# Attention, MLP and mixture of experts on one core: power-of-two scales in fewer links, and VectorE's work reordered around the weight scales, the first rows and the third gate chunk

## The chip, the core and the metric

The kernel runs on one core of a Trainium2 chip. The metric is the device time in microseconds (us) of that launch; the time of a kernel is the median of its runs.

## What is computed

```python
def phi(x):                                    # q, k: (4, 8, 576, 64), w_phi: (64, 128)
    proj = x @ w_phi
    proj = proj - max(abs(proj), axis=-1)
    return concat([exp(proj), exp(-proj)])     # 256 features
kv  = phi(k)^T @ v ;  z = sum over s of phi(k)
att = (phi(q) @ kv) / (phi(q) @ z + 1e-6)      # -> x: (2304, 512)
h = x @ w_in                                   # (512, 2048)
x = (h * clip(h + 3, 0, 6) / 6) @ w_out        # (2048, 512)
e = argmax(x @ w_gate)                         # 8 experts, one per row
out = softmax(x @ w_gate)[e] * sigmoid(x @ w_output_gate)[e] * (relu(x @ w1[e]) @ w2[e])   # (512, 1024, 512)
```

All inputs and outputs are fp32. The big products of the MLP and of the experts are made of fp16 parts: a matrix is scaled by a power of two, its high part is rounded to fp16, and its low part is what is left. Three matmuls (high*high, high*low, low*high) stand for one product. The power of two comes from the largest magnitude: its exponent bits are kept, the rest is masked away.

## The kernel before

The program is written engine by engine, with semaphores by hand. Each engine runs its own list in order, so a wait holds up all that stands behind it on that engine.

**Stage 1, attention (about 2.7 to 196 us).** The 32 heads are worked off as 16 pairs, u = 0 to 15. For each pair TensorE (PE) projects q and k in three groups (`projections`, L738, groups g0 of 4 matmuls, g1 and g2 of 16), VectorE (DVE) takes the maxima and the differences (`differences`, L1278, L1280, L1284), ScalarE (ACT) makes the exponentials (`k_features` L1088, `q_features` L1073), GpSimd (POOL) sums k's features (`sums_first` L587 three times, `sums_second` L587 and L603) and multiplies the result of an older pair by its reciprocals (`normalise`, L607), and PE makes kv (L766), z (L786), the numerators (L794) and the denominators (L803). A projection group of pair u+1 may only begin when `differences` has read the bank that it writes: g1 of pair u+2 waits for `differences(u+2, a, 0)`, g2 for `differences(.., 1)`.

DVE's list of a pair is `both(u, a, phase)`. Between the steps of the attention it does side work: `v_max` (L1312, largest magnitude of v of pair u+2), and, one eighth of w_in and of w_out per pair, in pairs 0 to 7 the search for the maximum (`piece_max_of`, L1317) and in pairs 8 to 15 the split (`piece_lo_of`: L1326 the high part of w_in, L1328 the low part of either; ACT's `piece_hi_of`, L1133, the high part of w_out).

**The two special pairs.** In pair 7 (`weights_pair`) the maxima of w_in, w_out and the gate weights are brought together: DVE reduces them (L1361, L1363), PE turns them over the partitions (`max_turn`, L810), DVE reduces again (L1344) and writes the result over a row (L1345, `s_rows`), and PE spreads it to all partitions (`max_over`, L814). Then `scales` makes the exponent, the reciprocal, the scale and its inverse (L1354 to L1357), each a link that waits for the one before. In pair 14 (`values_pair`) the same is done with the maximum of v for the rows x; then `first_x` writes the high part (L1439) and `x_lo` the low part (L1444) of the first 384 rows. DVE's list ends there with `piece_lo_of(14, 0, 1)`, the low part of a piece of w_out, and PE's first MLP block waits for it (`piece_lo`), beside `xs_lo` (the low part of the rows).

**Stage 2, MLP (197.5 to 584 us).** The 2304 rows go in 6 blocks of 384, each over 16 chunks f of the hidden width. PE: `hidden(n, a, f)` (12 matmuls, L878) runs two chunks ahead of `output(n, f)` (9 matmuls, L889). For each chunk ACT makes relu (L1216), DVE the product (`gate_chunk`, L1592), ACT the high part (L1227), DVE the low part (`gate_lo`, L1597); `output` waits for the low part. Where f is in SOON = (0, 1, 15), `gate_lo` stands right behind `gate_chunk`; else it is the last step of the chunk, behind the side work. The side work on DVE: 16 units of the experts' weights are searched (L1509), scaled (`unit_scale`, L1525 to L1529) and split (`unit_lo`, L1536), three units per block, and the rows of the block before are scaled (`row_scales` L1473 to L1482, `row_units` L1494 and L1495, `rows_lo` L1501) and routed.

**Stage 3, experts (584 to 850 us).** 27 slots of 128 rows: hidden (L972) and output (L984) on PE.

## Time and profile before

| | |
|---|---|
| time, median of 3 runs | 849.37 us (847.5 to 850.06) |
| the profiled execution, its own time | 852.16 us |
| span of the profiled execution | 850.5 us |
| busy: PE / DVE / ACT / POOL | 811.7 / 569.2 / 388.1 / 182.5 us |
| mean granted TensorE clock | 0.99 |

The span runs from the first to the last instruction of the profiled execution. Busy time of PE is modelled from pipelined matmuls, so a busy PE may still be waiting a little. Times of instructions below are microseconds from the start of the span.

### The profile page before, as it was taken

The numbers are of one execution on the slowest core, as the hardware profiler recorded it, in microseconds if no ns is written. First come the engines' busy times: TensorE is split into PE (matmuls) and PEld (weight loads), VectorE is DVE, ScalarE is ACT, GpSimd is POOL, SyncE is SP. The second block draws the span as 40 slices with busy tenths as digits, with TensorE's granted clock in tenths as the row PEclk, the third lists the DMA queues.
The fourth block names the chain that finished last, engine by engine and source line by source line (L and its number), as shares of the span: only waits on it lengthen the run. The fifth ranks groups of instructions, "written<-read, shape, count | busy, mean of one in ns | idle before, by whom it ended". The sixth has DMA issues, their size and how long they took to land.

```text
span 850.5 us, 19326 instructions
## 1 busy us (share of the span) xinstructions
PE 811.7 (95%) x7110; PEld 509.4 (60%) x7111; DVE 569.2 (67%) x1149; ACT 388.1 (46%) x841; POOL 182.5 (21%) x211
## 2 busy tenths in 40 slices
PE   6999999999999999999999999999889999999995
PEld 5666666665554554554555455556657777777773
DVE  4777878898988898897998998845622453222221
ACT  5777668884555646646546555524001121111110
POOL 4446547762000001001001001010220222111100
PEclk9999989999999999999999999999999999999998
DMA  7456647856564864955764855584171852556610
GB/s 229 150 186 206 201 139 226 234 160 212 198 243 149 241 238 162 267 205 187 243 225 185 247 209 210 150 293 178 51 278 47 322 207 84 222 225 218 222 69 14
DMA packets 67454, 164.41 MB, mean 193 GB/s; under 512 B 28615, under 2 KB 32967, under 8 KB 60737
## 3 DMA queue, kind: packets, MB, share of 16 engines
q1 hardware_dynamic: 61472, 146.74, 51.5%
q0 software_dynamic: 5760, 16.80, 5.7%
q8 instruction: 36, 0.59, 0.3%
q14 instruction: 26, 0.20, 0.1%
q10 hardware_dynamic: 160, 0.07, 0.0%
HBM read 114.16 MB, written 47.55 MB: 190 GB/s over the span
## 4 chain that ended last, share of the span: by engine, by line
PE 61%; DVE 23%; issue 8%; DMA 3%; ACT 2%; another core or an unknown queue 1%; DVEq 0%; POOL 0%; SPq 0%; ACTq 0%; POOLq 0%
PE ps L984 13%; PE ps L889 12%; PE ps L972 12%; PE ps L878 12%; DVE arena L1536 4%; PE ps L738 3%; DVE u_mx L1509 3%; DVE arena L1278 2%; PE ps L766 2%; PE ps L794 2%; DVE relu L1592 2%; DMA arena<-split 2%; PE ps L962 1%; DVE y_words L1501 1%; PE ps L752 1%
## 5 line engine op out<-in xcount | busy, mean ns | idle before, releaser
L878 PE MATMUL ps<-arena,w_in_sb 128*128 128x384 f16 x1152 | 200.9, 326 | 1.9 <-DVE w_out_sb L1328 1.9
L889 PE MATMUL ps<-w_out_sb,arena 128*128 128x512 f16 x576 | 171.3, 379 | 5.8 <-DVE stage L1597 5.8
L878 PEld LDWEIGHTS ps<-arena,w_in_sb 128*128 128x128 f16 x1152 | 111.9, 98 | 83.0 <-issue 2.1
L972 PE MATMUL ps<-x_t,arena 128*128 128x128 f16 x2112 | 121.5, 219 | 5.9 <-issue 5.9
L1255 ACT ACTIVATE x_t<-ps 128x512 f16<-128x512 f32 x54 | 31.6, 596 | 207.0 <-PE ps L972 176.1
L972 PEld LDWEIGHTS ps<-x_t,arena 128*128 128x128 f16 x2112 | 119.1, 98 | 10.2 <-issue 7.0
L984 PE MATMUL ps<-arena,x_t 128*128 128x512 f16 x528 | 118.0, 379 | 2.5 <-DVE x_t L1702 2.5
L889 PE MATMUL ps<-w_out_sb,stage 128*128 128x512 f16 x288 | 109.1, 379 | 0.0
L1227 ACT ACTIVATE arena<-relu 128x384 f16<-128x384 f32 x96 | 50.0, 521 | 114.1 <-DVE relu L1592 114.1
L1088 ACT ACTIVATE arena<-ps,arena 128x128 f32<-128x128 f32 x288 | 79.9, 393 | 34.8 <-DVE arena L1280 27.8
L889 PEld LDWEIGHTS ps<-w_out_sb,arena 128*128 128x128 f16 x576 | 55.6, 98 | 67.0 <-issue 8.6
L1702 DVE SCALAR_TENSOR_TENSOR x_t<-ps,x_t 128x512 f16<-128x512 f32 x54 | 36.7, 689 | 85.6 <-ACT x_t L1255 85.6
L1216 ACT ACTIVATE relu<-ps,three,s_h 128x384 f32<-128x384 f32 x96 | 63.7, 663 | 56.7 <-PE ps L878 55.2
L984 PEld LDWEIGHTS ps<-arena,x_t 128*128 128x128 f16 x528 | 50.5, 98 | 59.4 <-ACT x_t L1255 2.9
L1536 DVE SCALAR_TENSOR_TENSOR arena<-arena,u_up 128x1024 f16<-128x1024 f32 x64 | 79.3, 1280 | 6.3 <-ACT arena L1204 5.6
L587 POOL TENSOR_TENSOR arena<-arena 128x512 f32<-128x512 f32 (+1 forms) x64 | 64.5, 1008 | 71.8 <-ACT arena L1088 67.3
L1204 ACT ACTIVATE arena<-arena,u_up 128x1024 f16<-128x1024 f32 x64 | 72.5, 1140 | 6.5 <-DVE u_up L1528 6.3
L1509 DVE TENSOR_REDUCE u_mx<-arena 128x1 f32<-128x1024 f32 x64 | 74.8, 1210 | 0.0
L636 POOL PARTITION_ALL_REDUCE u_all<-u_red x16 | 7.6, 476 | 307.1 <-DVE u_red L1513 307.1
L1592 DVE SCALAR_TENSOR_TENSOR relu<-relu,ps 128x384 f32<-128x384 f32 x96 | 52.7, 549 | 26.1 <-ACT relu L1216 24.4
L1278 DVE TENSOR_REDUCE arena<-ps 128x8 f32<-128x1024 f32 (+1 forms) x48 | 45.8, 954 | 35.5 <-PE ps L738 35.3
L1712 DVE TENSOR_SCALAR x_t<-ps,stage 128x512 f32<-128x512 f32 x27 | 20.2, 748 | 70.0 <-PE ps L984 70.0
(208 smaller groups left out, 931.0 us busy)
## 6 DMA issues: line engine op xcount, KB each, us to landing
arena<-split SPq DMA_DIRECT2D x36, 1024.0 KB
arena<-in_moe_w SPq DMA_DIRECT2D x16, 2048.0 KB
split<-arena SPq DMA_DIRECT2D x16, 2048.0 KB, 7.4
arena<-in_qkt SPq DMA_DIRECT2D x15, 576.0 KB, 6.7
stage<-in_moe_w_in SPq DMA_DIRECT2D x16, 512.0 KB, 5.3
stage<-in_moe_w_out SPq DMA_DIRECT2D x16, 512.0 KB, 6.5
x_t<-rows POOLq DMA_DIRECT2D x27, 257.0 KB, 3.0
y_words<-recs SPq DMA_DIRECT2D x32, 144.0 KB, 3.1
```

Of the source, the lines that this page charges most:

```text
L587: nc.gpsimd.tensor_tensor(out, x, y, ALU.add).then_inc(sum_step, 1)
L878: last = nc.tensor.matmul(ps[:, HB[f % GB], 0:BN], w_in_sb[:, lw, c, f * P:(f + 1) * P], xt[:, a, lx, c, :], start=c == 0 and lw + lx == 0 ...
L889: last = nc.tensor.matmul(ps[:, YB + r, :], g_sb[lg_][:, f % GB, r * P:(r + 1) * P], w_out_sb[:, lw, f, :], start=f == 0 and lg_ + lw == 0 ...
L972: last = nc.tensor.matmul(ps[:, bank, f % 4 * P:(f % 4 + 1) * P], w1_sb[b][:, lw, c, f * P:(f + 1) * P], xgt[:, a, lx, c, :], start=c == 0 ...
L984: last = nc.tensor.matmul(ps[:, 6 + a, :], hg[:, a, lh, f, :], w2_sb[b][:, lw, f, :], start=f == 0 and lh + lw == 0, stop=f == EFC - 1 and ...
L1088: last = nc.scalar.activation(pk[:, t0 + t, s, :], ps[:, bank, t * F:(t + 1) * F], ACT.Exp, bias=bias[:, t0 + t:t0 + t + 1], scale=1.0 - 2 ...
L1204: nc.scalar.activation(split_sb[:, 0, q_ * Q:(q_ + 1) * Q], raw[b][:, q_ * Q:(q_ + 1) * Q], ACT.Copy, scale=u_up[:, b:b + 1]).then_inc(u_h ...
L1216: nc.scalar.activation(relu3[:, f % GB, :], ps[:, HB[f % GB], 0:BN], ACT.Relu, bias=three[:, 0:1], scale=s_h[:, 0:1]).then_inc(relu3_ready, 1)
L1278: nc.vector.tensor_reduce(mx[:, j:j + 2, t0:t0 + n], src, AX.X, ALU.max, apply_absolute_value=True).then_inc(max_ready, 1)
L1509: nc.vector.tensor_reduce(u_mx[:, q_:q_ + 1], raw[b][:, q_ * Q:(q_ + 1) * Q], AX.X, ALU.max, apply_absolute_value=True).then_inc(u_searche ...
L1536: nc.vector.scalar_tensor_tensor(out=split_sb[:, 1, cols], in0=raw[b][:, cols], scalar=u_up[:, b:b + 1], in1=split_sb[:, 0, cols], op0=ALU ...
L1592: nc.vector.scalar_tensor_tensor(out=relu3[:, f % GB, :], in0=relu3[:, f % GB, :], scalar=6.0, in1=ps[:, HB[f % GB], 0:BN], op0=ALU.min, o ...
```

## The change

- **Scales in three links.** `scales`, `row_scales` and `unit_scale` made the power of two in clamp, mask, reciprocal, multiply (and inverse). Now they mask, then clamp and multiply to the inverse scale in one instruction, then take its reciprocal as the scale. The inverse scales hold the factor that was multiplied in later, so two later multiplications (that of `slot_inv` for the early slots, and L1783) become a copy or nothing.
- **No spread row.** The copy to `s_rows` (L1345) is gone; PE reads `s_row` as a broadcast.
- **The maxima pair.** In `weights_pair` the gate weights' maximum is taken first, the search of the w_out piece moves behind `differences(u + 1, 1 - a, 1)`, and `scales` comes ahead of `v_max`, which moves behind `differences(u + 2, a, 0)`. In `both`, `v_max` also moves behind `differences(u + 2, a, 0)`.
- **First rows.** In `values_pair`, `first_x` comes ahead of the steps to `s_h` and `s_y` (`x_units`). PE's first block no longer waits for the last piece of w_out (a semaphore of its own, `piece_lo_out`). POOL's last two `normalise` wait for `xs_lo`.
- **MLP blocks.** SOON also holds 2. `row_units` moves from f = 0 to f = 4.

```diff
-USTEPS = 5
+USTEPS = 4
-SOON = (0, 1, FC - 1)
+SOON = (0, 1, 2, FC - 1)
...
             def last_pair():
                 sums_second(PAIRS - 1)
+                pool.wait_ge(xs_lo, 1)
                 for u in range(PAIRS - 1 - BEHIND, PAIRS - LAST):
                     normalise(u, u % 2)
...
                     pe.wait_ge(piece_hi, PAIRS // 2 - 1)
-                    pe.wait_ge(piece_hi_out, PAIRS // 2 - 1)
                     pe.wait_ge(piece_lo, PAIRS // 2 - 1)
+                    pe.wait_ge(piece_hi_out, PAIRS // 2 - 2)
+                    pe.wait_ge(piece_lo_out, PAIRS // 2 - 2)
...
             def max_over_rows(k, n):
                 dve.wait_ge(max_turned, k + 1)
-                scaled(nc.vector.tensor_reduce(s_row[0:n, :], ps[0:n, KVB, 0:P], AX.X, ALU.max))
-                nc.vector.tensor_copy(s_rows[0:n, :], s_row[0:n, :].to_broadcast([n, P])).then_inc(max_spread, 1)
+                nc.vector.tensor_reduce(s_row[0:n, :], ps[0:n, KVB, 0:P], AX.X, ALU.max).then_inc(max_spread, 1)
 
             def max_of(k, cols):
                 dve.wait_ge(num_done, TOPS[k] + 1)
-                scaled(nc.vector.tensor_scalar(s_max[:, cols], ps[:, NB + 1, MAX_AT:MAX_AT + (cols.stop - cols.start)], TINY, None, ALU.max))
+                top = ps[:, NB + 1, MAX_AT:MAX_AT + (cols.stop - cols.start)]
+                scaled(nc.vector.tensor_scalar(s_pow[:, cols].bitcast(I32), top.bitcast(I32), EXPONENT, None, ALU.bitwise_and))
 
             def scales(cols):
-                scaled(nc.vector.tensor_scalar(s_pow[:, cols].bitcast(I32), s_max[:, cols].bitcast(I32), EXPONENT, None, ALU.bitwise_and))
-                scaled(nc.vector.reciprocal(s_up[:, cols], s_pow[:, cols]))
-                scaled(nc.vector.tensor_scalar(s_up[:, cols], s_up[:, cols], 2.0 ** TOP, None, ALU.mult))
-                scaled(nc.vector.tensor_scalar(s_inv[:, cols], s_pow[:, cols], 2.0 ** -TOP, None, ALU.mult))
+                scaled(nc.vector.tensor_scalar(s_inv[:, cols], s_pow[:, cols], TINY, 2.0 ** -TOP, ALU.max, ALU.mult))
+                scaled(nc.vector.reciprocal(s_up[:, cols], s_inv[:, cols]))
...
             def both(u, a, phase):
                 differences(u + 1, 1 - a, 2)
                 pair_out(u, a)
-                v_max(u + 2, a)
                 piece(u, a, 1)
                 differences(u + 2, a, 0)
+                v_max(u + 2, a)
 
             def weights_pair():
                 u, a = TOPS[0], 1
-                for w in range(2):
-                    piece_max_of(u, a, w)
+                gate_max()
+                piece_max_of(u, a, 0)
+                differences(u + 1, 1 - a, 1)
+                piece_max_of(u, a, 1)
                 weight_max()
-                differences(u + 1, 1 - a, 1)
                 max_over_rows(0, 3)
                 differences(u + 1, 1 - a, 2)
                 max_of(0, slice(0, 3))
                 pair_out(u, a)
+                scales(slice(0, 3))
+                differences(u + 2, a, 0)
                 v_max(u + 2, a)
-                weight_scales()
-                differences(u + 2, a, 0)
...
                 pair_out(u, a)
-                x_scales()
+                scales(slice(3, 4))
                 first_x()
+                x_units()
                 piece_lo_of(u, a, 1)
...
-                link(nc.vector.tensor_scalar(y_mx[:], y_mx[:], TINY, None, ALU.max))
                 link(nc.vector.tensor_scalar(y_pow[:].bitcast(I32), y_mx[:].bitcast(I32), EXPONENT, None, ALU.bitwise_and))
-                link(nc.vector.reciprocal(y_up[:], y_pow[:]))
-                link(nc.vector.tensor_scalar(y_up[:], y_up[:], 2.0 ** ETOP, None, ALU.mult))
+                link(nc.vector.tensor_scalar(y_inv[:], y_pow[:], TINY, 2.0 ** -ETOP, ALU.max, ALU.mult))
+                link(nc.vector.reciprocal(y_up[:], y_inv[:]))
...
-                link(nc.vector.tensor_scalar(u_all[:, b:b + 1], u_all[:, b:b + 1], TINY, None, ALU.max))
-                link(nc.vector.tensor_scalar(pow_.bitcast(I32), u_all[:, b:b + 1].bitcast(I32), EXPONENT, None, ALU.bitwise_and))
-                link(nc.vector.reciprocal(u_up[:, b:b + 1], pow_))
-                link(nc.vector.tensor_scalar(u_up[:, b:b + 1], u_up[:, b:b + 1], 2.0 ** ETOP, None, ALU.mult))
-                link(nc.vector.tensor_copy(u_pow[:, bass.ds(u, 1)], pow_))
+                link(nc.vector.tensor_scalar(u_pw[:, b:b + 1].bitcast(I32), u_all[:, b:b + 1].bitcast(I32), EXPONENT, None, ALU.bitwise_and))
+                link(nc.vector.tensor_scalar(u_inv[:, b:b + 1], u_pw[:, b:b + 1], TINY, 2.0 ** -ETOP, ALU.max, ALU.mult))
+                link(nc.vector.reciprocal(u_up[:, b:b + 1], u_inv[:, b:b + 1]))
+                nc.vector.tensor_copy(u_unit[:, bass.ds(u, 1)], u_inv[:, b:b + 1]).then_inc(u_step, 1)
...
                     if f == 0 and post:
+                        unit_lo(n * 3 - 1, 1 - a, 2)
+                    if f == 4 and post:
                         row_units(n - 1)
-                        unit_lo(n * 3 - 1, 1 - a, 2)
```

## Rows read from the trace of the kernel before

**Rows 1.** The page: TensorE's granted clock in 40 slices, in tenths.
```profile
PEclk9999989999999999999999999999999999999998
```

**Rows 2.** Timeline of PE, pair 7: start, us, engine, line, what, idle before.
```profile
97.95 1.16 PE L738 MATMUL ps<-wphi_sb,arena 64*128 64x128 f32 x16 [1.01 <-DVE arena L1284]
...
108.56 1.16 PE L738 MATMUL ps<-wphi_sb,arena 64*128 64x128 f32 x16 [2.01 <-DVE arena L1284]
109.65 1.41 PE L786 MATMUL ps<-ones,arena 128*128 128x1 f32 x8
...
117.15 1.19 PE L803 MATMUL ps<-arena 128*32 128x144 f32 x32
```

**Rows 3.** Windows: stretch, length, busy (instructions) by engine, clock, DMA share, GB/s.
```profile
113.00:115.00 2.00, 2.00 (x18) 1.69 (x16) 0.91 (x1) 1.48 (x3) 1.49 (x1) 0.50 0.64 229
```

**Rows 4.** Timeline of PE, an ordinary pair of the second half.
```profile
156.80 1.16 PE L738 MATMUL ps<-wphi_sb,arena 64*128 64x128 f32 x16 [0.26 <-DVE arena L1284]
157.89 1.05 PE L786 MATMUL ps<-ones,arena 128*128 128x1 f32 x8
...
162.21 1.19 PE L803 MATMUL ps<-arena 128*32 128x144 f32 x32
```

**Rows 5.** Timeline of DVE, pair 7.
```profile
103.59 0.81 DVE L1312 TENSOR_REDUCE v_mx<-arena 128x1 f32<-128x640 f32 x1
...
105.13 1.11 DVE L1356 TENSOR_SCALAR s_up<-s_up 128x3 f32<-128x3 f32 x1
106.28 1.32 DVE L1357 TENSOR_SCALAR s_inv<-s_pow 128x3 f32<-128x3 f32 x1
```

**Rows 6.** Timeline of POOL: first half, pair 7, second half.
```profile
80.81 1.27 POOL L603 TENSOR_TENSOR arena<-arena 128x512 f32<-128x512 f32 x1
...
106.17 1.40 POOL L607 TENSOR_TENSOR x_t<-x_t,y_words 128x576 f32<-128x576 f32 x1
...
154.98 2.13 POOL L603 TENSOR_TENSOR arena<-arena 128x512 f32<-128x512 f32 x1
```

**Rows 7.** Timeline of ACT, the ordinary pair of the second half.
```profile
157.22 0.63 ACT L1088 ACTIVATE arena<-ps,arena 128x128 f32<-128x128 f32 x2 [1.18 <-POOL arena L603]
```

**Rows 8.** Timeline of DVE, pairs 14 and 15, and the same x_lo later.
```profile
184.95 1.13 DVE L1345 COPY s_rows<-s_row 1x128 f32<-1x128 f32 x1
...
190.30 1.86 DVE L1439 TENSOR_SCALAR arena<-x_t,s_up 128x1536 f16<-128x1536 f32 x1
192.19 2.85 DVE L1444 SCALAR_TENSOR_TENSOR arena<-x_t,s_up,arena 128x1536 f16<-128x1536 f32 x1
194.97 2.43 DVE L1328 SCALAR_TENSOR_TENSOR w_out_sb<-stage,s_up,w_out_sb 128x1024 f16<-128x1024 f32 x1
...
233.31 1.82 DVE L1444 SCALAR_TENSOR_TENSOR arena<-x_t,s_up,arena 128x1536 f16<-128x1536 f32 x1
```

**Rows 9.** Timeline of PE, pair 15 and the start of the MLP.
```profile
189.66 1.08 PE L766 MATMUL ps<-arena 128*64 128x256 f32 x8 [0.81 <-ACT arena L1088]
...
197.54 2.76 PE L878 MATMUL ps<-arena,w_in_sb 128*128 128x384 f16 x16 [1.87 <-DVE w_out_sb L1328]
```

**Rows 10.** Timeline of PE's weight loads and matmuls, blocks 1 and 2.
```profile
322.66 0.13 PEld L889 LDWEIGHTS ps<-w_out_sb,arena 128*128 128x128 f16 x2 [0.73 <-ACT arena L1227]
...
339.35 0.13 PEld L889 LDWEIGHTS ps<-w_out_sb,arena 128*128 128x128 f16 x2 [1.31 <-issue]
...
343.27 0.59 PE L889 MATMUL ps<-w_out_sb,arena 128*128 128x512 f16 x2
```

**Rows 11.** Timeline of DVE, start of block 2.
```profile
326.76 0.17 DVE L1479 TENSOR_SCALAR y_mx<-y_mx 128x3 f32<-128x3 f32 x1
...
328.84 0.56 DVE L1597 SCALAR_TENSOR_TENSOR stage<-relu,arena 128x384 f16<-128x384 f32 x1 [0.59 <-ACT arena L1227]
...
329.97 2.48 DVE L1536 SCALAR_TENSOR_TENSOR arena<-arena,u_up 128x1024 f16<-128x1024 f32 x2 [0.17 <-DVE y_log L1495]
...
342.06 0.55 DVE L1597 SCALAR_TENSOR_TENSOR stage<-relu,arena 128x384 f16<-128x384 f32 x1
```

More of the change, by code:

```diff
@@ L65 @@
 Q = UW // 4
-USTEPS = 5
+USTEPS = 4
 Y_AT = 3
 UNIT_AT = 1
-SOON = (0, 1, FC - 1)
-X_UP = 11
-YSTEPS, YUP = 7, 5
+SOON = (0, 1, 2, FC - 1)
+W_UP = 3
+YSTEPS, YUP = 6, 4
 ONEHOT, ARGS, ROUTE = 6, 8, 21
@@ L173, in moe_program @@
         s_red = sb("s_red", [P, 4])
-        s_max = sb("s_max", [P, 4])
         s_row = sb("s_row", [3, 1])
-        s_rows = sb("s_rows", [3, P])
         s_pow = sb("s_pow", [P, 4])
@@ L185, in moe_program @@
         warm = sb("warm", [P, 1])
-        u_pow = sb("u_pow", [P, UNITS])
+        u_unit = sb("u_unit", [P, UNITS])
         u_pw = sb("u_pw", [P, 2])
+        u_inv = sb("u_inv", [P, 2])
         u_up = sb("u_up", [P, 2])
@@ L190, in moe_program @@
         y_pow = sb("y_pow", [P, BT])
+        y_inv = sb("y_inv", [P, BT])
         y_up = sb("y_up", [P, BT])
@@ L263, in moe_program @@
         piece_lo = sem("piece_lo")
+        piece_lo_out = sem("piece_lo_out")
         scale_step = sem("scale_step")
@@ L268, in moe_program @@
         piece_hi_out = sem("piece_hi_out")
-        w_scale = sem("w_scale")
         x_scale = sem("x_scale")
@@ L440, in next_pieces @@
                 else:
-                    sp.wait_ge(piece_lo, u - PAIRS // 2 + 1)
+                    sp.wait_ge(piece_lo_out, u - PAIRS // 2 + 1)
                 load_pieces(piece // 2, u % 2, piece)
@@ L813, in max_over @@
                 pe.wait_ge(max_spread, k + 1)
-                nc.tensor.matmul(ps[:, NB + 1, MAX_AT:MAX_AT + n], s_rows[0:n, :], ident[0:n, 0:n], start=True, stop=True).then_inc(num_done, 1)
+                nc.tensor.matmul(ps[:, NB + 1, MAX_AT:MAX_AT + n], s_row[0:n, :].to_broadcast([n, P]), ident[0:n, 0:n], start=True, stop=True).then_inc(num_done, 1)
             def both(u, a, more=True, top=None):
@@ L941, in mlp_block @@
                         pe.wait_ge(piece_hi, PAIRS // 2)
+                        pe.wait_ge(piece_lo, PAIRS // 2)
                         pe.wait_ge(piece_hi_out, PAIRS // 2)
-                        pe.wait_ge(piece_lo, PAIRS // 2)
+                        pe.wait_ge(piece_lo_out, PAIRS // 2)
                     if f + 2 < FC:
@@ L1129, in piece_hi_of @@
             def piece_hi_of(u, a):
-                act.wait_ge(w_scale, 1)
+                act.wait_ge(scale_step, W_UP)
                 act.wait_ge(stage_loaded[a], (u - a) * 16 + 32)
@@ L1200, in unit_hi @@
                 if q_ == 0:
-                    act.wait_ge(u_step, u * USTEPS + 4)
+                    act.wait_ge(u_step, u * USTEPS + 3)
                     if not isinstance(u, int) or u > 0:
@@ L1329, in piece_lo_of @@
                                                       in1=dst[:, 0, cols], op0=ALU.mult, op1=ALU.subtract)
-                if w == 1:
-                    done.then_inc(piece_lo, 1)
+                done.then_inc((piece_lo, piece_lo_out)[w], 1)
             scale_steps = [0]
@@ L1388, in weights_pair @@
                 pair_out(u, a)
+                scales(slice(0, 3))
+                assert scale_steps[0] == W_UP
+                differences(u + 2, a, 0)
                 v_max(u + 2, a)
-                weight_scales()
-                differences(u + 2, a, 0)
             def values_pair():
@@ L1428, in x_max, with x_units @@
                 nc.vector.tensor_reduce(s_red[:, 3:4], v_mx[:], AX.X, ALU.max).then_inc(max_in, 1)
-            def x_scales():
-                scales(slice(3, 4))
-                assert scale_steps[0] == X_UP + 1
+            def x_units():
                 scaled(nc.vector.tensor_tensor(s_h[:], s_inv[:, 3:4], s_inv[:, 0:1], ALU.mult))
@@ L1492, in link @@
                     dve.wait_ge(row_step, n * YSTEPS + at[0])
-                link(nc.vector.tensor_scalar(y_den[:], y_pow[:], s_y[:, 0:1], 2.0 ** -ETOP, ALU.mult, ALU.mult))
+                link(nc.vector.tensor_scalar(y_den[:], y_inv[:], s_y[:, 0:1], None, ALU.mult))
                 link(nc.vector.tensor_scalar(y_log[:], y_den[:], s_inv[:, 2:3], None, ALU.mult))
@@ L1615, in star_pick @@
                 nc.vector.tensor_scalar(star_i[:], star1[:, 1:2], float(E), None, ALU.add).then_inc(star_ready, 1)
-                nc.vector.tensor_tensor(e_inv[:], u_pow[:].rearrange("p (e m) -> p e m", m=2)[:, :, 0],
-                                        u_pow[:].rearrange("p (e m) -> p e m", m=2)[:, :, 1], ALU.mult)
+                dve.wait_ge(u_step, UNITS * USTEPS)
+                nc.vector.tensor_tensor(e_inv[:], u_unit[:].rearrange("p (e m) -> p e m", m=2)[:, :, 0],
+                                        u_unit[:].rearrange("p (e m) -> p e m", m=2)[:, :, 1], ALU.mult)
                 starred(nc.vector.tensor_tensor(star8[:, 0], iota8[:, 0, :], star1[:, 1:2].to_broadcast([P, E]), ALU.is_equal))
@@ L1622, in star_pick @@
                 starred(nc.vector.tensor_reduce(star1[:, 3:4], star8[:, 2], AX.X, ALU.add))
-                starred(nc.vector.tensor_scalar(slot_inv[:, 0:EARLY], star1[:, 3:4].to_broadcast([P, EARLY]), 2.0 ** (-2 * ETOP), None, ALU.mult))
+                starred(nc.vector.tensor_copy(slot_inv[:, 0:EARLY], star1[:, 3:4].to_broadcast([P, EARLY])))
             def early_rows():
@@ L1782, in _ @@
             link(nc.vector.tensor_reduce(slot_inv[:, EARLY:SLOTS], sl[:, 2], AX.X, ALU.add))
-            link(nc.vector.tensor_scalar(slot_inv[:, EARLY:SLOTS], slot_inv[:, EARLY:SLOTS], 2.0 ** (-2 * ETOP), None, ALU.mult))
             def slot(s, a, turn, more=True):
```

9 lines of the change are left out of this document (3 added, 6 removed).

## The prediction, made before the changed kernel was run

> **What bounds the kernel now.** I read the page first: TensorE (PE) is granted nearly full speed throughout, but one slice of 40, the sixth, shows 8 tenths [rows 1]. Then I read the chain of waits from end to end. It is PE's in pairs 0 to 6, DVE's from pair 7 to the start of the MLP, PE's in the MLP except around the start and the end of each block, where it passes through DVE, and PE's among the experts. So only PE's own gaps are for sale, and I looked each of them up in the timelines.
>
> Pair 7 has two: g2 of the next projections waits 1.01 us for the differences, g1 waits 2.01 us [rows 2]. Right behind the second, the same work takes longer: from L786 to L803 it is 109.65 to 117.15, 7.50 us, where an ordinary pair takes 157.89 to 162.21, 4.32 us [rows 2, 4]. In that stretch the granted clock is 0.50, the lower level, 1.2 GHz in place of 2.4 [rows 3]. The ordinary pairs of the second half wait 0.26 us each [rows 4]. At the end of the attention PE waits 0.81 us for ACT, then 1.87 us for the low part of a w_out piece before the first MLP matmul [rows 9]. In the MLP it waits 1.31 us in front of output(2), which needs DVE's low half of chunk 2, and 0.73 us in front of output(15) [rows 10]. The first of these stands in all five blocks after block 0, the second in the first four of them.
>
> **The change, part by part.**
>
> *Pair 7.* DVE's differences for g1 end just before 108.56. Ahead of them it now does the copy to s_rows (as in pair 14, 1.13 us), v_max 0.81, and the links L1356 with 1.11 and L1357 with 1.32 [rows 5, 8]. The change takes out the copy and one of the two long links and moves v_max behind: 3.05 us. PE reached g1 at 108.56 - 2.01 = 106.55. The first wait goes as well: one search and two reductions are moved behind the differences that g2 needs. Then PE is at g1 1.01 earlier, at 105.54, and DVE, which waits for g2 in between, ends its differences at 108.5 - 1.01 - 3.05 = 104.4. Both waits are gone with 1.1 us to spare: 3.02 us. With the gaps the fall of the clock should go, since everything else in that pair is as in its neighbours: 7.50 - 4.32 = 3.18 us. What is behind v_max now: only the next differences, which wait for PE anyway, so it is hidden. What the moved w_out search is late for is PE's max_turn, behind g2: nothing, or a tenth. Bounds of this part: 3.0 (the clock falls all the same) to 6.2. I take 6.2.
>
> The Trainium skill (TensorE: Matmul & The Clock Gate, "HAM oscillation") blames longer gaps of PE than the two here for such a fall. By it the cause would be another one, and the 3.18 us might stay; the trace, where the fall follows directly on the wait and no pair without it has one, speaks against that. It is a rival below.
>
> *Ordinary pairs.* v_max (0.81) leaves DVE's path to g1, which is late by only 0.26. Seven pairs by 0.26 would be 1.8 us. But ACT's next k exponentials wait 1.18 us for POOL's L603 in the same pair [rows 7], and that L603 takes 2.13 us where it takes 1.27 in the first half [rows 6]: it stands behind DVE's low part of w_out. ACT and POOL form a closed round there that is as long as DVE's. DVE will issue that low part earlier, but the delay then falls on the POOL instruction before. So PE will wait for ACT instead of DVE: I take 0, and keep 1.8 as the other end. A loss I exclude, as each DVE step is as early or earlier.
>
> *Pair 14 and the first rows.* The copy (1.13) is gone, so ACT's exponentials start earlier and PE's 0.81 wait goes. first_x starts earlier by the copy, two links and the three steps to s_y. x_lo takes 2.85 us beside POOL's normalise and 1.82 without [rows 8]; POOL now waits, so 1.03 less. The low part is then ready at 195.04 - 1.13 - 1.03 = 192.9 or before. PE ends its attention at 197.54 - 1.87 - 0.81 = 194.9: it no longer waits, and the w_out piece (2.43) is off its path. Gain 0.81 + 1.87 = 2.7 us, if PE itself sets the start; bounds 2.0 and 3.0.
>
> What that queues: POOL's two normalise, 1.40 each [rows 6], now meet x_units and the w_out piece, and behind them stands DVE's first gate_chunk. Nothing waits for those normalise until chunk 7. In block 0 DVE was the later one by a little in front of output(1); I charge 0.2 us, at most 1.5. SP's loads of the first units follow the end of the attention and come earlier with it.
>
> The Trainium skill (SBUF — State Buffer, "Who interferes with whom") says that DVE and POOL exclude each other for a whole instruction where DVE has two SBUF inputs or runs a fast one-input mode. The trace agrees: L1357, three numbers a row, ends at 107.60, with POOL's L607 at 107.57 [rows 5, 6].
>
> *MLP blocks.* At a block's start one link (0.17, some 0.2 with its wait) goes ahead of chunk 0, and row_units no longer stands between 328.84 + 0.56 = 329.40 and 329.97 [rows 11]. So DVE is 0.2 + 0.57 = 0.77 us earlier at chunks 1 and 2. output(2) then no longer waits. The price: with f = 2 in SOON, gate_lo(2) stands right behind gate_chunk(2) and must wait for ACT, 0.59 as for chunk 0 [rows 11]. gate_lo(3) comes at 342.06 - 0.77 + 0.59 = 341.88, ends at 342.43, and PE can begin output(3) at about 342.55. PE, freed of its 1.31, is there at 343.27 - 1.31 = 341.96 [rows 10]. It waits 0.6 us: 1.31 becomes 0.6, one chunk later. row_units at f = 4 costs 0.57, but unit_scale behind it is a link shorter and waits for POOL's maximum anyway; nothing late. Towards the end of the block DVE follows PE's pace and gains one more link in unit_scale, in the chain unit_scale, ACT's unit_hi, relu(15): 0.2 off the 0.73. Together 0.9 us in four blocks and 0.7 in the last: 4.3. Bounds: 1.5 (output(3) takes over most of the wait) to 6.5 (neither wait left at chunks 2 and 3).
>
> *End.* One link of the last row_scales is on the path to the last transposes: 0.2. The multiplication left out in the slots' table has nobody waiting.
>
> **Sum.** 6.2 + 0 + 2.7 - 0.2 + 4.3 + 0.2 = 13.2 us off the profiled execution's 852.16, so 839.0 there. That execution is 2.8 us above the median of 849.37; against the median I predict 836.2.
>
> **Rivals.**
> - *The clock falls all the same* in the attention: 3.2 us stay, 839.4. For it: only one such fall is in the trace, so its cause rests on one case. Chance 0.10.
> - *The block's wait only moves*: DVE is busy without a pause over chunks 1 to 4, and if gate_lo(3) is as late as gate_lo(2) was, only the links' 0.2 and 0.2 per block remain, 2 of 4.3: 838.5, with the last pieces of block 0 late as well 840. Chance 0.13.
> - *POOL's two normalise hit DVE before the first chunk* and block 0 pays 1.5: 837.5. Chance 0.06.
> - *The ordinary pairs gain too*: 1.8 more, 834.4. Against it: ACT's wait for POOL. Chance 0.08.
> - *Slower*: the clock. A block now has a wait at output(3) and one at output(15). If they bring about a fall as in pair 7, each costs 3.2 us; in five blocks 16 us, and the sum turns to 852.2. It decides from five falls on. Against it: the same blocks hold 1.31 and 0.73 now at full clock. Chance 0.03.
> - *It does nothing*: the waits in pair 7 and before the MLP were set by something later than DVE, such as the piece loads, and the gain shrinks to under 2.5 us. Chance 0.02.
>
> My forecast has the remaining 0.58. The time is 836.2. Range: from 832.8 (ordinary pairs 1.8, and a larger gain in the blocks) to 841.5 (the clock's 3.2 with half the gain of the blocks). Changes under 0.3%, 2.5 us, can't be told from none here. Faster by more: 0.95; within: 0.02; slower: 0.03.
>
> **What would show it.** In the changed profile: all slices at 9, no PE gap over 0.3 us in pairs 7 and 8, and L786 to L803 of pair 8 near 4.3 us; ordinary pairs still 0.3 us over PE's own work, with PE now waiting for ACT in front of L794; no gap before the first L878 and x_lo at about 1.8; in the blocks no wait before output(2), about 0.6 before output(3) and 0.5 before output(15). I am wrong if the sixth slice still shows 8, if gate_lo(3) is later than 0.6 after PE, or if the first gate_chunk of block 0 comes much later after the first matmul than 2.9 us.

## The result: 849.1 to 836.5 us

| | before | after |
|---|---|---|
| median | 849.11 us (847.5 to 850.06, 4 runs) | 836.46 us (835.14 to 837.7, 4 runs) |
| the profiled execution, its own time | 852.16 us | 835.77 us |
| span, granted clock | 850.5 us, 0.99 | 834.1 us, 0.995 |

The ratio is 0.985, with a 95% interval of 0.9827 to 0.9872: 1.5% faster. Predicted were 836.2 us and a range of 832.8 to 841.5. Line numbers of the kernel after differ a little from those of before (L803 is L804, L786 is L787, L889 is L890, L1444 is L1443, L1328 is L1331, L1597 is L1593).

From the page of the kernel after: the granted clock in 40 slices, and the chain of waits by engine.

```profile
PEclk9999999999999999999999999999999999999998
...
PE 76%; DVE 8%; POOL 5%; ACT 4%; issue 4%; DMA 2%; ACTq 0%; DVEq 0%; POOLq 0%
```

The sixth slice, an 8 before [rows 1], is a 9. PE's share of the chain was 61% and DVE's 23%; now DVE carries 8%. The view of PE's waits says the same by line (us in total, times, longest): first before, then after.

```profile
PE ps L889 <- DVE stage L1597: 5.8, 10, 1.1
...
PE ps L738 <- DVE arena L1284: 4.3, 7, 2.0
...
PE ps L878 <- DVE w_out_sb L1328: 1.9, 1, 1.9
PE ps L766 <- ACT arena L1088: 0.8, 1, 0.8
```

```profile
PE ps L795 <- ACT arena L1107: 1.4, 6, 0.3
PE ps L890 <- DVE stage L1593: 1.3, 5, 0.3
PE ps L787 <- issue: 0.5, 1, 0.5
```

PE's timeline after, in three places: pairs 7 and 8 (both groups of 16 projections without a wait, and L787 to L804 in 4.32 us at full clock, where [rows 2] had 7.50), an ordinary pair (a wait for ACT in place of that for DVE in [rows 4]), and the start of the MLP (no wait, against [rows 9]).

```profile
97.58 1.16 PE L739 MATMUL ps<-wphi_sb,arena 64*128 64x128 f32 x16
...
106.15 1.16 PE L739 MATMUL ps<-wphi_sb,arena 64*128 64x128 f32 x16
107.24 1.05 PE L787 MATMUL ps<-ones,arena 128*128 128x1 f32 x8
...
111.56 1.19 PE L804 MATMUL ps<-arena 128*32 128x144 f32 x32
...
164.83 1.30 PE L795 MATMUL ps<-arena 128*64 128x320 f32 x8 [0.25 <-ACT arena L1107]
...
185.68 1.02 PE L787 MATMUL ps<-ones,arena 128*128 128x1 f32 x8 [0.46 <-issue]
...
189.85 6.03 PE L879 MATMUL ps<-arena,w_in_sb 128*128 128x384 f16 x36
```

The weight loads of the MLP after: what comes before output(3) and output(15), in blocks 1 and 2. They answer to [rows 10]; in front of output(2) nothing is left.

```profile
270.07 0.13 PEld L890 LDWEIGHTS ps<-w_out_sb,arena 128*128 128x128 f16 x2 [0.62 <-issue]
...
313.82 0.15 PEld L890 LDWEIGHTS ps<-w_out_sb,arena 128*128 128x128 f16 x2 [0.28 <-issue]
...
333.72 0.13 PEld L890 LDWEIGHTS ps<-w_out_sb,arena 128*128 128x128 f16 x2 [0.61 <-issue]
...
377.46 0.14 PEld L890 LDWEIGHTS ps<-w_out_sb,arena 128*128 128x128 f16 x2 [0.29 <-issue]
```

A ledger of the two profiled executions, cut at instructions that both have:

| stretch | before | after | gained | predicted |
|---|---|---|---|---|
| start to pair 8's L803 | 117.15 | 111.56 | 5.6 | 6.2 |
| pairs 9 to 14, to pair 14's L803 | 68.07 | 68.25 | -0.2 | 0 |
| from there to the first MLP matmul | 12.32 | 10.04 | 2.3 | 2.7 |
| block 0, to the first matmul of block 1 | 62.30 | 62.30 | 0.0 | -0.2 |
| blocks 1 to 5 | 324.5 | 319.2 | 5.3 | 4.3 |
| the rest | 266.1 | 262.7 | 3.4 | 0.2 |

The first row holds 0.7 us of start-up the other way: the first L803 comes at 21.88 us before and at 22.58 after. Most of the last row is no work of the change either: in the execution of before, ACT stood still in stage 3 for something that the chain names no engine for, and PE with it for 2.5 us; this execution of after doesn't have this. The view of the chain of before has it in one line (start, length, what):

```profile
602.00 5.53 another core or an unknown queue
```

Without the start-up and the last row the profiles differ by 13.7 us, where the sum had 13.0 for these rows; the medians differ by 12.65.

One profile isn't the kernel's average, though. The same code profiled again (e13, below) has the pause, and its last row takes 269.3 us, 6.6 more than this one; over all fourteen profiles, PE's work in it being the same in each, it is 262.8 to 269.8. Its block 0 takes 64.7 us and not 62.3. The profile of after is a favourable one in both stretches; e13's own time is 843.47 us (on another chip), 7.7 above its 835.77.

### The profile page after: what moved, and what is told of

Read it like the earlier page. It is cut to its first block, busy times and chain, and to the rows that moved or that the text cites. A ratio compares the mean times of both kernels' runs of the same rounds, so it can differ in the third digit from the quotient of the medians.

```text
span 834.1 us, 19259 instructions
## 1 busy us (share of the span) xinstructions
PE 807.9 (97%) x7110; PEld 508.1 (61%) x7111; DVE 559.6 (67%) x1119; ACT 387.0 (46%) x841; POOL 180.1 (22%) x211
## 4 chain that ended last, share of the span: by engine, by line
PE 76%; DVE 8%; POOL 5%; ACT 4%; issue 4%; DMA 2%; ACTq 0%; DVEq 0%; POOLq 0%
PE ps L890 19%; PE ps L879 17%; PE ps L987 13%; PE ps L975 13%; POOL arena L587 4%; PE ps L767 3%; PE ps L739 3%; PE ps L795 3%; DVE u_mx L1507 2%; ACT arena L1091 2%; DMA arena<-split 2%; PE ps L753 2%; DVE y_words L1499 1%; DVE arena L1532 1%; PE ps L804 1%
## 5 line engine op out<-in xcount | busy, mean ns | idle before, releaser
L890 PE MATMUL ps<-w_out_sb,arena 128*128 128x512 f16 x576 | 171.4, 379 | 1.3 <-DVE stage L1593 1.3
L890 PE MATMUL ps<-w_out_sb,stage 128*128 128x512 f16 x288 | 109.3, 379 | 0.0
L890 PEld LDWEIGHTS ps<-w_out_sb,arena 128*128 128x128 f16 x576 | 55.6, 98 | 61.6 <-issue 4.5
L587 POOL TENSOR_TENSOR arena<-arena 128x512 f32<-128x512 f32 (+1 forms) x64 | 69.4, 1084 | 65.2 <-ACT arena L1091 60.0
```

The lines of the kernel that those rows point to most:

```text
L587: nc.gpsimd.tensor_tensor(out, x, y, ALU.add).then_inc(sum_step, 1)
L890: last = nc.tensor.matmul(ps[:, YB + r, :], g_sb[lg_][:, f % GB, r * P:(r + 1) * P], w_out_sb[:, lw, f, :], start=f == 0 and lg_ + lw == 0 ...
```

## Experiments

Twelve runs in three groups, the last of them the kernel after once more. Within a group all ran on one chip in the same rounds, with the kernel before among them. The chips differ a little (before: 848.98, 854.61 and 851.81 us), so ratios to before are compared across groups. One execution differs from the next by some 0.5%; effects of 1 to 3 us are therefore read in the traces, between two instructions that both kernels have.

### The second wait and the clock

**e1: the old order in pair 7, all else as after** (group 1)

```diff
+                for w in range(2):
+                    piece_max_of(u, a, w)
                 gate_max()
-                piece_max_of(u, a, 0)
+                weight_max()
                 differences(u + 1, 1 - a, 1)
-                piece_max_of(u, a, 1)
-                weight_max()
...
+                v_max(u + 2, a)
                 scales(slice(0, 3))
...
                 differences(u + 2, a, 0)
-                v_max(u + 2, a)
```

> The changed kernel, with the old order of steps in pair 7 alone (both searches and the reductions ahead of the differences for g2, v_max and then the scales ahead of the differences for g1); the copy to s_rows stays out and the scales keep three links. My theory counts microseconds on VectorE: the 1.01 us wait before g2 comes back, the wait before g1 does not (0.81 us of v_max return of 3.05 us taken out, with 1.1 us to spare), and the clock stays up. So about 1.0 us slower than the changed kernel, 837.5 us, with no granted clock under 1.0 in pair 8. Rival: the order, not the copy and the link, carries the gain of the pair; then both waits and the fall of the clock are back and it is about 6 us slower, 842.6 us.

Measured: 839.63 us (837.15 to 841.19), ratio 0.9877 (0.9843 to 0.991). Its PE timeline in pair 7:

```profile
97.03 1.98 PE L739 MATMUL ps<-wphi_sb,arena 64*128 64x128 f32 x16 [1.05 <-DVE arena L1287]
```

The wait in front of g2 is back with 1.05 us, none in front of g1. But the clock, which was expected to stay up, fell right there, at this wait of 1 us alone: the same 16 projections took 1.98 us in place of 1.16, and the windows view has 0.52 and 0.64 granted in the 4 us from 97.10 on. From pair 7's L787 to pair 8's L804 it took 93.70 to 112.33 = 18.6 us, after 95.37 to 111.56 = 16.2: some 1.0 us of wait and 1.4 of low clock.

**e2: only pair 7's order, put into the kernel before** (group 1)

```diff
-                for w in range(2):
-                    piece_max_of(u, a, w)
+                gate_max()
+                piece_max_of(u, a, 0)
+                differences(u + 1, 1 - a, 1)
+                piece_max_of(u, a, 1)
                 weight_max()
-                differences(u + 1, 1 - a, 1)
...
-                v_max(u + 2, a)
                 weight_scales()
                 differences(u + 2, a, 0)
+                v_max(u + 2, a)
```

> The kernel before, with the new order of steps in pair 7 alone (gate maximum first, the w_out search behind the differences for g2, the scales ahead of v_max, v_max behind the differences for g1); the copy and the four links stay. My theory: the 1.01 us wait before g2 goes, the 2.01 us wait before g1 falls to about 1.1. If a wait of that length alone does not let the clock fall, the gain is 1.0 + 0.9 + 3.2 = 5.1 us, about 844.0 us. Rival: the clock falls after any wait at that place; then the gain is 1.9 us, about 847.2 us, and the granted clock is 0.50 again in pair 8.

Measured: 845.21 us (843.31 to 849.26), ratio 0.9954 (0.9932 to 0.9976). Neither wait is left and all slices of the clock are 9, though the copy to `s_rows` and the fourth link are still there. I had expected 1.1 us in front of g1. DVE's timeline of e2 in pair 7:

```profile
99.21 0.91 DVE L1345 COPY s_rows<-s_row 3x128 f32<-3x128 f32 x1
...
103.17 0.91 DVE L1356 TENSOR_SCALAR s_up<-s_up 128x3 f32<-128x3 f32 x1
104.12 0.17 DVE L1357 TENSOR_SCALAR s_inv<-s_pow 128x3 f32<-128x3 f32 x1
```

```profile
102.76 1.30 POOL L587 TENSOR_TENSOR arena<-arena 128x512 f32<-128x512 f32 x1 [1.12 <-ACT arena L1088]
104.14 1.28 POOL L603 TENSOR_TENSOR arena<-arena 128x512 f32<-128x512 f32 x1
```

The second fence is POOL's timeline of e2. L1356 ends at 104.08, with L587 (104.06). L1357 takes 0.17 us here, where it took 1.32 [rows 5]: DVE got to it between POOL's two instructions. So much of the links' cost in pair 7 was not theirs: it was POOL's instruction beside them, and the order took the larger of the two. The other stayed: L1356 has 0.91 us here, and in the kernel after the one tensor_scalar that is left in that place has 0.96. The order is enough for the second wait, and so (e1) is the removal of the copy and the link: that gain has two causes, each of which suffices. Only the order takes the first.

**e6: a wait made in front of g1** and **e7: the same in front of g2 and g1** (group 2). The line `filler(3, 1)` is in e7 alone.

```diff
+            def filler(c0, n):
+                for c in range(c0, c0 + n):
+                    nc.vector.tensor_reduce(fill[:, c:c + 1], ident[:, None, :].to_broadcast([P, 8, P]), AX.XY, ALU.max)
...
+                filler(3, 1)
                 differences(u + 1, 1 - a, 1)
...
+                filler(0, 3)
                 differences(u + 2, a, 0)
```

> Adds to the kernel after three reductions of the identity (8x128 elements a row, some 1.2 us each) on VectorE in pair 7, ahead of the differences that g1 needs, to no purpose but the time they take. PE then waits some 2 us in front of g1, as in the kernel before, and not in front of g2. Theory: that wait alone brings the clock down to 0.50 from L786 to L803 of pair 8 (7.5 us in place of 4.3): 2.0 + 3.2 = 5.2 us longer than the kernel after. Rival one: it takes both waits, and the clock stays up: 2.0 us longer. Rival two: the fall has nothing to do with the waits, and the same follows, 2.0 us, with 4.3 us for the stretch.

> The kernel of e6_wait_g1 with one more such reduction ahead of the differences that g2 needs, so that PE waits some 1 us in front of g2 and some 2 us in front of g1, as in the kernel before. Theory: the stretch from L786 to L803 of pair 8 takes 7.5 us at 0.50, and the sum is 1.0 + 2.0 + 3.2 = 6.2 us longer than the kernel after. Rival: the fall had another cause than the waits; then the stretch takes 4.3 us at full clock and the sum is 3.0.

Measured: e6 844.26 us (842.16 to 848.7), ratio 0.9885 (0.9849 to 0.9922); e7 846.64 us (843.88 to 850.14), ratio 0.9908 (0.9872 to 0.9944). The kernel after has 0.985, and by the medians of the same rounds e6 is 3.0 us and e7 5.4 us above e5, which by its trace is the kernel after within a us. PE's timeline of e6, then the windows view of e6 over the same stretch (per engine busy us and instructions, then granted clock, DMA share and GB/s):

```profile
106.87 1.16 PE L740 MATMUL ps<-wphi_sb,arena 64*128 64x128 f32 x16 [1.82 <-DVE arena L1288]
107.96 1.23 PE L788 MATMUL ps<-ones,arena 128*128 128x1 f32 x8
...
111.45 2.08 PE L740 MATMUL ps<-wphi_sb,arena 64*128 64x128 f32 x16
115.37 1.23 PE L805 MATMUL ps<-arena 128*32 128x144 f32 x32
```

```profile
104.00:106.00 2.00, 1.05 (x8) 0.62 (x6) 2.00 (x2) 0.37 (x1) 1.07 (x1) 1.00 0.07 17
106.00:108.00 2.00, 1.13 (x17) 1.01 (x17) 1.51 (x5) 1.35 (x5) 0.00 (x0) 1.00 0.46 140
108.00:110.00 2.00, 2.00 (x14) 1.64 (x14) 1.86 (x3) 1.84 (x6) 0.00 (x0) 0.67 0.82 223
110.00:112.00 2.00, 2.00 (x10) 0.79 (x8) 1.84 (x3) 2.00 (x8) 0.19 (x1) 0.50 0.93 319
112.00:114.00 2.00, 2.00 (x20) 1.59 (x18) 0.62 (x2) 0.77 (x1) 1.92 (x2) 0.50 0.39 135
114.00:116.00 2.00, 2.00 (x28) 1.04 (x28) 1.71 (x4) 0.94 (x4) 0.88 (x2) 0.62 0.64 55
```

One wait of 1.82 us, made by DVE work that has no other effect, is followed by the clock's lower level, 1.2 GHz, though PE is busy without a pause from 106.87 on. By the shares of the first and the last of the low windows it lasted from about 108.7 to 115.5, some 7 us. L788 to L805 takes 107.96 to 115.37 = 7.41 us; after has 4.32. From pair 7's L811 to the first MLP matmul, e6 needs 97.73 to 193.89 = 96.16 us, after 98.91 to 189.85 = 90.94: 5.2 us, the number expected, though some 0.5 of it is a longer wait for ACT in two ordinary pairs, which e5 has in four. By the medians it is 3.0 us, with intervals that hold 5. In e7 the waits are 0.82 and 1.83 us and the pair's stretch is 5.8 us longer than after, 22.0 against 16.2; before had 22.5. The rival that the fall has nothing to do with the wait falls: in this place a wait made on purpose brings it about. In other places it need not: the wait of 1.87 us in front of before's first MLP matmul [rows 9] was followed by no fall (granted 1.00 from 194 to 204 us).

### The first rows

**e3: the first rows behind the last piece again** (group 1)

```diff
-                pool.wait_ge(xs_lo, 1)
...
-                    pe.wait_ge(piece_hi_out, PAIRS // 2 - 2)
-                    pe.wait_ge(piece_lo_out, PAIRS // 2 - 2)
+                    pe.wait_ge(piece_hi_out, PAIRS // 2 - 1)
+                    pe.wait_ge(piece_lo_out, PAIRS // 2 - 1)
...
+                x_units()
                 first_x()
-                x_units()
```

> The changed kernel, with the first rows undone: TensorE's first MLP block waits again for the last low part of a w_out piece, GpSimd's last two normalise do not wait for xs_lo, and the three steps to s_y come ahead of first_x again. My theory: the first MLP matmul comes when that low part ends, near 192 us in place of 189.9, so about 2.1 us slower, 838.6 us, and TensorE waits about 2 us there. Rival: in the changed kernel TensorE's own attention work sets the start so closely that the order hardly matters, under 0.7 us slower.

Measured: 837.32 us (834.57 to 839.31), ratio 0.9849 (0.9812 to 0.9886): the median shows no difference to after's 0.985. In the trace the wait is back:

```profile
190.54 6.01 PE L878 MATMUL ps<-arena,w_in_sb 128*128 128x384 f16 x36 [1.89 <-DVE w_out_sb L1330]
```

From pair 7's L811 (97.29) that is 93.25 us, after 90.94: 2.3 us more. But 0.9 of it is a longer wait for ACT in four ordinary pairs, which e5 has too and which has nothing to do with this part. From pair 14's L804 on, e3 takes 179.12 to 190.54 = 11.4 us, after 179.81 to 189.85 = 10.0: 1.4 us are this part's, between the 2.1 expected and the rival's 0.7, and below what the medians resolve. It is less than the wait of 1.89, since PE's 0.46 in front of L787 isn't there in e3.

### The blocks

**e4: SOON and `row_units` as before, links as after** (group 1) and **e5: SOON as before alone**, the diff's first two lines (group 2)

```diff
-SOON = (0, 1, 2, FC - 1)
+SOON = (0, 1, FC - 1)
...
                     if f == 0 and post:
+                        row_units(n - 1)
                         unit_lo(n * 3 - 1, 1 - a, 2)
-                    if f == 4 and post:
-                        row_units(n - 1)
```

> The changed kernel, with SOON = (0, 1, FC - 1) again and row_units back at f = 0; the links stay out. My theory: in each of the five blocks after block 0 TensorE waits about 1.1 us before output(2) (1.31 less one link) and nothing before output(3), in place of 0.61 before output(3): 0.5 us per block, 2.5 us in all, about 839.0 us. Rival: the block's wait hardly depends on this order, and the links made the gain of the blocks: under 1 us slower, 837.3 us.

> Of the kernel after, chunk 2 is taken out of SOON alone: step 2's low half of chunk 2 again stands behind the next chunk's work; row_units stays moved and the links stay three. By my theory the 0.77 us that DVE gained at chunks 1 and 2 leaves a wait of 1.31 - 0.77 = 0.5 us in front of output(2) and none in front of output(3), where the kernel after has none and 0.6: the same time within 0.5 us. Rival: chunk 2 in SOON carries the blocks' gain, the wait in front of output(2) is back at 1.1 or more, and the time is 2.5 us longer than that of the kernel after.

Measured: e4 841.05 us (839.57 to 842.52), ratio 0.9897 (0.9864 to 0.993); e5 841.24 us (840.23 to 843.34), ratio 0.9847 (0.9816 to 0.9878). In front of output(2) of block 2, e4 and then e5; in front of output(3) neither waits:

```profile
332.11 0.13 PEld L890 LDWEIGHTS ps<-w_out_sb,arena 128*128 128x128 f16 x2 [1.10 <-issue]
```

```profile
331.31 0.13 PEld L890 LDWEIGHTS ps<-w_out_sb,arena 128*128 128x128 f16 x2 [0.44 <-issue]
```

The period of a block, from one output(15) to the next (block 1 to 2), sorts the parts:

| | before | e4 | after | e5 | e9, below |
|---|---|---|---|---|---|
| links | 4 | 3 | 3 | 3 | 3 |
| `row_units` at f = | 0 | 0 | 4 | 4 | 4 |
| chunk 2's low half | late | late | at once | late | between |
| period, us | 64.70 | 64.14 | 63.64 | 63.47 | 63.22 |

The links give 0.56 us a block, `row_units` with SOON 0.50. SOON's new entry alone costs 0.17: of the three edits for the blocks it is the one that doesn't pay. These differences are small but clear: with one and the same code (after, e13) the period is 63.64 us both times. Both expectations held in the blocks: over all five, e4 is 2.4 us longer than after (2.5 expected) and e5 0.8 shorter. That e4's ratio is 0.0047 above after's, 4 us, is not the blocks alone: its block 0 is 1.8 us longer, for the reason shown under e8.

**e9: the low half of chunk 2 between the two reductions of the search** (group 3)

```diff
-SOON = (0, 1, 2, FC - 1)
+SOON = (0, 1, FC - 1)
...
-            def unit_search(u, b, q0):
+            def unit_search(u, b, q0, between=None):
...
+                    if between is not None and q_ == q0 + 1:
+                        between()
...
-                        unit_search(n * 3 + k, (a + k) % 2, 0)
+                        unit_search(n * 3 + k, (a + k) % 2, 0, (lambda: gate_lo(n, 2)) if f == 2 else None)
...
-                    if f not in SOON:
+                    if f not in SOON and f != 2:
```

> Of the kernel after, in every block step 2's low half of chunk 2 goes between the two reductions of the unit search that stands behind it, in place of ahead of both. Theory: the 0.6 us wait in front of output(3) is DVE's wait for ACT's high half of chunk 2 passed on; behind one reduction of 1.2 us nothing is waited for, output(2) has the time (in the kernel after it doesn't wait), and 5 blocks by 0.6 = 3.0 us go. Rival: the low half is then late for output(2) by as much, and the 0.6 only moves back one chunk: no change.

Measured: 840.96 us (838.26 to 841.29), ratio 0.9854 (0.9831 to 0.9878); the kernel after beside it (e13, below) 0.9849. DVE's timeline of e9 at chunks 2 and 3 of block 1: L1595, the low half, waits for nothing, where a low half right behind its product waits 0.59 for ACT [rows 11].

```profile
263.13 0.55 DVE L1590 SCALAR_TENSOR_TENSOR relu<-relu,ps 128x384 f32<-128x384 f32 x1
263.59 1.21 DVE L1509 TENSOR_REDUCE u_mx<-arena 128x1 f32<-128x1024 f32 x1
264.72 0.55 DVE L1595 SCALAR_TENSOR_TENSOR stage<-relu,arena 128x384 f16<-128x384 f32 x1
265.19 1.21 DVE L1509 TENSOR_REDUCE u_mx<-arena 128x1 f32<-128x1024 f32 x1
```

All five waits in front of output(3) are gone, and from the first MLP matmul to L902 e9 takes 188.05 to 576.08 = 388.0 us, e13 188.60 to 578.91 = 390.3: 2.3 us, not the 3.0 expected, since a weight load stands some 0.2 us idle in front of an output even when nobody is late. The medians don't show the 2.3 us; the traces do.

### The ordinary pairs, and where a gain was given back

**e8: the w_out piece behind v_max and g1's differences in the ordinary pairs** (group 2)

```diff
-                piece(u, a, 1)
-                differences(u + 2, a, 0)
-                v_max(u + 2, a)
+                if phase:
+                    v_max(u + 2, a)
+                    differences(u + 2, a, 0)
+                    piece(u, a, 1)
...
```

> Of the kernel after, in the ordinary pairs of the second half DVE's w_out piece is put behind v_max and the differences for g1. Theory: POOL's L587 and L603, which ACT's exponentials wait for, are then not held by the piece's low part; the pairs go from 11.34 to PE's own 11.0, six by 0.3, 1.9 us shorter than the kernel after. Rival: the piece then holds another of POOL's instructions in the same round, and the pairs stay at 11.3: no change. The other end: DVE is late for g2 by a part of the piece's 1.8 us, and each pair loses up to 0.8, 5 us.

Measured: 840.77 us (837.85 to 843.97), ratio 0.9841 (0.9805 to 0.9877). POOL and ACT in an ordinary pair: first after, where ACT waits 1.28 us for POOL's L603 behind 5.11 us of L587, then e8.

```profile
168.07 5.11 POOL L587 TENSOR_TENSOR arena<-arena 128x512 f32<-128x512 f32 x4 [3.53 <-ACT arena L1091]
...
174.63 0.62 ACT L1091 ACTIVATE arena<-ps,arena 128x128 f32<-128x128 f32 x2 [1.28 <-POOL arena L603]
```

```profile
154.88 4.50 POOL L587 TENSOR_TENSOR arena<-arena 128x512 f32<-128x512 f32 x4 [2.82 <-ACT arena L1091]
159.47 1.27 POOL L603 TENSOR_TENSOR arena<-arena 128x512 f32<-128x512 f32 x1
160.70 2.39 POOL L607 TENSOR_TENSOR x_t<-x_t,y_words 128x576 f32<-128x576 f32 x1
...
160.85 0.63 ACT L1091 ACTIVATE arena<-ps,arena 128x128 f32<-128x128 f32 x2 [0.32 <-POOL arena L603]
```

The delay that DVE's w_out piece causes POOL is now on L607, which nobody waits for (2.39 us in place of 1.4), and the pair takes PE's own 11.02 us in place of 11.33. From L811 to the first MLP matmul: 98.64 to 187.53 = 88.89 us, 2.05 us less than after. But block 0 gave back more than that. ACT and PE at its start, in e8:

```profile
192.90 0.67 ACT L1219 ACTIVATE relu<-ps,three,s_h 128x384 f32<-128x384 f32 x1 [4.29 <-DMA rows<-relu]
...
195.46 0.59 PE L890 MATMUL ps<-w_out_sb,arena 128*128 128x512 f16 x2 [1.90 <-DVE stage L1598]
...
200.52 0.59 PE L890 MATMUL ps<-w_out_sb,arena 128*128 128x512 f16 x2 [1.01 <-DVE stage L1598]
```

The zero rows for the experts' gather are stored by DMA from the tile that relu later writes, eight stores on SP's queue, the last one in pair 15 (L462). SP issued it at 188.98. ACT was done with its work before at 188.61 and went on at 192.90; in e11, below, the same wait is 1.08 us and for PE. The kernel after meets the same store: in its own profile ACT's relu waits 1.08 us and for PE only, but in e13, the same code, 3.49 us for this DMA. Most of the profiled executions have this wait: of the eight whose start of the MLP is that of the kernel after (after, e1, e4 to e7, e9, e13), five do, and their block 0 takes 63.4 to 64.7 us where the other three have 62.3. e2, the kernel before with its attention 5 us shorter, has it too (63.4); before itself doesn't (62.3).

**e11: e8 with the last store issued one pair earlier; e12: e8, e9 and e11 together; e13: the kernel after, unchanged** (group 3)

```diff
-                if e >= 0:
+                for e in ([e] if 0 <= e < E - 2 else [E - 2, E - 1] if e == E - 2 else []):
                     sp.dma_start(rows[e * REGION:e * REGION + P, :], zrow).then_inc(pads_stored, 16)
```

> The kernel of e8_piece_behind, with the last of the eight stores of zero rows issued one pair earlier on SP's queue, with the one before it. In e8's trace PE reached the MLP 2.05 us earlier, from pair 7's L804, and then waited 1.90 us in front of output(0) and 1.01 us in front of output(1) of block 0, behind ACT's first relu, which waited 4.29 us for that store. Theory: the store is what gave the gain back. Both waits go, 2.9 us shorter than e8_piece_behind and 2 us shorter than the kernel after. Rival: DVE's pieces are late for chunk 1 anyway, and 1 us of wait stays.

> The edits of e8_piece_behind, e9_lo_between and e11_pads_early together. The three are in different stretches, so by my theory they add: 2.0 and 3.0 us, 5 us shorter than the kernel after, 0.6%. Rival: as for each of them, 2 to 3 us.

> The kernel after, unchanged, beside the three versions, so that they are compared with it in the same rounds. The ratio to the kernel before should be 0.985 again. Whether its ordinary pairs wait 0.25 or 0.5 us for ACT differed between the other runs: both were seen with this same code.

Measured, with the stretches of the traces:

| | e13 (after) | e9 | e11 | e12 |
|---|---|---|---|---|
| median, us | 840.08 (837.37 to 843.47) | 840.96 | 839.13 (835.86 to 840.94) | 835.9 (834.58 to 838.94) |
| ratio to before | 0.9849 (0.9821 to 0.9876) | 0.9854 | 0.9834 (0.9807 to 0.9861) | 0.9812 (0.9786 to 0.9839) |
| L811 to first MLP matmul | 91.02 | 90.92 | 89.44 | 88.86 |
| first MLP matmul to L902 | 390.31 | 388.03 | 387.91 | 385.75 |

ACT's first relu, e13 and then e11:

```profile
193.17 0.67 ACT L1219 ACTIVATE relu<-ps,three,s_h 128x384 f32<-128x384 f32 x1 [3.49 <-DMA rows<-relu]
```

```profile
190.08 0.67 ACT L1219 ACTIVATE relu<-ps,three,s_h 128x384 f32<-128x384 f32 x1 [1.08 <-PE ps L879]
```

The earlier store takes 2.4 us out of the MLP (390.31 to 387.91), e9's edit 2.2 (387.91 to 385.75), e8's 2.2 out of the attention (1.6 in e11): 6.7 us between e13's trace and e12's up to L902. Against the first profile of after, which didn't wait for the store (387.89), it is 4.2 us, and of the medians it is 4.2 us as well. The two ratios' intervals overlap slightly, so the exact size stays open; e12 has the lowest ratio of all versions, 1.9% under the kernel before.

## Why the prediction was right

**Pair 7 and the clock** (6.2 predicted): right. From pair 6's L803 to pair 8's it is 29.18 us before and 22.88 after, 6.3 less. Both waits went, and 4.32 us for L787 to L804 is the predicted 4.3. e6 shows the cause: a wait of 1.82 us brings the fall, 3.1 us of price. Two things in my working were too simple. I summed copy, link and v_max to 3.05 us in front of g1; e2 shows that the order alone removes the wait, because v_max is out of the way and the longest link was held by POOL. And I tied the fall to the second wait; e1 shows that one of 1.05 us can do it as well. The Trainium skill (TensorE: Matmul & The Clock Gate, "HAM oscillation") blames longer gaps of PE; here, by e6, one of 1.82 us was enough in this place, so the rival drawn from it falls.

**Ordinary pairs** (0): -0.2, a small loss where I had excluded one (pair 9 now waits 0.17 us for ACT), but with the mechanism named: POOL's delay moved from L603 (2.13 before, 1.26 us after) to L587, ACT waits 1.28 us, PE 0.25. The 1.8 us kept as the other end were there for the taking, but needed another order (e8).

**Pair 14 and the first rows** (2.7): 2.3. x_lo was to take 1.82 us; it took 2.71, since POOL's L603 of the last pair (1.87 us), not its `normalise`, ran beside it. DVE was early enough all the same. The missing 0.4 is PE's new wait of 0.46 in front of L787. The view names no engine for it; L603 ends at 185.59, 0.09 before PE goes on, so it is probably that L603, which I had not followed into pair 15. e3 shows that the first rows' own edit is worth 1.4 of the 2.3.

**Blocks** (4.3): 5.3, the size a little low, each step as told: no wait at output(2), 0.6 at output(3), as computed. Under-sized was the term "one more link in unit_scale, 0.2": output(15) went from 0.73 to 0.28 us, so the links give 0.56 a block, not 0.4. And chunk 2 in SOON, which I counted as part of the gain, costs 0.17 (e5). The larger part of the excess is a thing that I hadn't seen: I took all blocks as alike, but in before the one from output(15) of block 2 to that of block 3 takes 65.33 us where its neighbours take 64.69, with a further wait, in front of output(1). After has 63.65 there as elsewhere. The last block gained 0.4 and not 0.7.

```profile
399.43 0.13 PEld L889 LDWEIGHTS ps<-w_out_sb,arena 128*128 128x128 f16 x2 [0.58 <-issue]
```

**Block 0** (-0.2): 0.0 in the profile of after, but -1.1 to -2.4 us in five of the other seven with the same start. The rival had `normalise` in front of the first chunk; that didn't come. What does come is ACT's wait for the store of zero rows. It was no term of my sum, and that step was missing: the change lets the MLP start before that store has landed.

**The rest**: my 0.2 at L902 is there (0.78 to 0.57 us of wait). Of the other 3.2 us of the profiles 2.5 are that one pause of ACT, which nine of the fourteen profiles have and five, after's first among them, don't. Taking the median as the base and not the profile kept the 2.8 us between them out of the forecast; that they are this pause isn't shown.

**The number.** That 836.2 came so near to 836.46 is in part luck. In the rows of the sum the profile has 0.7 us more than I had (13.7 against 13.0), from +1.0 in the blocks and -0.4 in the first rows, and block 0 gives back 1 to 2.4 us in most executions, for which the sum had 0.2.

## What to carry to other kernels

Find the waits of PE that are followed by a low clock: removing 3 us of waiting gave back 6. When a short instruction is long in the trace, look at what another engine runs at that moment before counting it as a cost; moving it may do more than removing it. And a gain in one stage lands on whatever the next stage had ready only just in time: look there for stores that free a buffer, as e8 and e11 did.

## What the hardware showed unexpectedly

- The clock doesn't always fall at the wait: in e1 it was down in the 2 us behind it, in e6 PE first worked at full clock for about 2 us. The low level lasted some 3.5 us in e1 and some 7 in e6 and before. A wait of 1.05 us brought a fall in e1, one of 1.01 (before, in front of g2) and one of 0.82 us (e7) brought none at once, nor did one of 1.87 at the start of before's MLP. The length of a single wait doesn't decide alone.
- In stage 3 PE's weight loads stand idle for 4.0 us in the profiles of before and of after (e11's PE waits there for the DMA of the experts' weights), and the 96 matmuls behind it run at full clock (5.36 us of weight loads in both). In all twelve runs above the same wait, of 3.7 to 4.5 us, goes with a fall, and those loads take 6.7 to 7.8 us. One and the same code had either outcome (after, e13). The pause of 2.5 us in stage 3 likewise: behind it the clock fell in six of the nine profiles that have it. The line of e13:

```profile
627.45 6.98 PEld L975 LDWEIGHTS ps<-x_t,arena 128*128 128x128 f16 x96 [4.16 <-issue]
```

- A tensor_scalar of DVE on 3 numbers a row takes 0.15 to 1.32 us, by what POOL runs beside it; the reciprocal of the same three took 0.16 to 0.18 in before, after and e2, in e2 in the middle of POOL's L587 (102.96 against 102.76 to 104.06).
- The last DMA store of 257 KB landed 3.4 us behind its issue in after's profile and 4.4 us in e13's, with the same code. A buffer that is free just in time in one execution is late in the next.
